# Moving one MLP tile between the score and the state products of a linear-attention output

## The reference

```python
for t in range(S):
    cur = np.einsum('bhd,bhe->bhde', u[None] * kt, vt)
    y[:, :, t] = np.einsum('bhd,bhde->bhe', rt, state + cur)
    state = wt[:, :, :, None] * state + np.einsum('bhd,bhe->bhde', kt, vt)
...
h = x @ w_in
g = np.where(h > 0.0, h, alpha * (np.exp(np.minimum(h, 0.0)) - 1.0))
x = g @ w_out
...
h = x @ w_in2
out = (h * (1.0 / (1.0 + np.exp(-1.702 * h)))) @ w_out2
```

## Time and profile before

| | |
|---|---|
| median of 3 runs | 1036.31 us (1035.52 to 1036.63) |
| profiled execution, its time | 1033.64 us |
| profiled execution, its span | 1031.5 us |
| TensorE busy | 953.8 us, 92% |
| VectorE busy | 548.6 us, 53% |
| ScalarE busy | 456.4 us, 44% |
| mean granted TensorE clock | 0.973 |
| the seven riding steps | about 90 to 573 us from the start |

### The profile page before, as it was taken

The page is one execution under the profiler, slowest core; times in us unless marked ns, Lnnn a source line. Parts: engine busy times, 40 slices in busy tenths (PEclk is TensorE's granted clock), DMA queues, the critical chain, the costliest instruction groups (busy, mean ns, idle before and its releaser), DMA issues.

```text
span 1031.5 us, 27033 instructions
## 1 busy us (share of the span) xinstructions
PE 953.8 (92%) x11872; PEld 922.7 (89%) x11872; DVE 548.6 (53%) x900; ACT 456.4 (44%) x859; POOL 54.0 (5%) x62
## 2 busy tenths in 40 slices
PE   3647999999989999999999999999999999999998
PEld 3537989888988889899888999999999999999998
DVE  7758558567477566585574443443343433443333
ACT  2343643644634635536445576333333333333332
POOL 2011000000000000000000164000000000000000
PEclk8567999999999999999999999999999999999999
DMA  6154121130130211211200651000000000000000
GB/s 167 43 142 116 25 54 48 25 87 15 31 95 7 68 51 25 54 48 24 58 22 2 216 176 44 1 24 1 23 0 24 0 23 0 23 0 24 1 24 24
DMA packets 15413, 47.29 MB, mean 46 GB/s; under 512 B 2864, under 2 KB 6832, under 8 KB 15312
## 3 DMA queue, kind: packets, MB, share of 16 engines
q1 hardware_dynamic: 12720, 38.21, 13.1%
q0 software_dynamic: 1952, 6.81, 2.1%
q10 hardware_dynamic: 640, 0.72, 0.3%
HBM read 35.71 MB, written 8.85 MB: 43 GB/s over the span
## 4 chain that ended last, share of the span: by engine, by line
PE 82%; DVE 9%; issue 4%; ACT 3%; DMA 1%; DVEq 0%; ACTq 0%
PE psum L1089 37%; PE psum L1102 34%; PE psum L941 4%; DVE blocks L667 2%; DVE arena L613 2%; PE psum L1043 1%; DVE arena L580 1%; ACT expo L411 1%; PE psum L1002 1%; PE psum L903 1%; ACT expo L409 1%; PE psum L950 1%; PE psum L1038 1%; DVE gate L713 1%; DVE x_lo L700 1%
## 5 line engine op out<-in xcount | busy, mean ns | idle before, releaser
L1089 PE MATMUL psum<-x_hi,w_split 128*128 128x384 f32 x1536 | 395.6, 338 | 1.0 <-issue 1.0
L1102 PE MATMUL psum<-g_hi,w_split 128*128 128x384 f32 x1536 | 393.2, 337 | 0.0
L1089 PE MATMUL psum<-x_lo,w_split 128*128 128x384 f32 x768 | 264.9, 345 | 21.2 <-DVE x_lo L700 19.3
L1089 PEld LDWEIGHTS psum<-x_hi,w_split 128*128 128x128 f32 x1536 | 281.9, 189 | 1.2 <-issue 1.1
L1102 PEld LDWEIGHTS psum<-g_hi,w_split 128*128 128x128 f32 x1536 | 278.5, 189 | 0.0
L1102 PE MATMUL psum<-g_lo,w_split 128*128 128x384 f32 x768 | 262.0, 341 | 0.0
L420 ACT ACTIVATE g_hi<-gate 128x384 fp32r<-128x384 f32 x256 | 134.5, 525 | 169.5 <-DVE gate L713 87.0
L718 DVE TENSOR_TENSOR g_lo<-gate,g_hi 128x384 fp32r<-128x384 f32 x256 | 142.8, 558 | 124.1 <-ACT g_hi L420 123.4
L1089 PEld LDWEIGHTS psum<-x_lo,w_split 128*128 128x128 f32 x768 | 144.9, 189 | 25.9 <-DVE x_lo L700 15.2
L711 DVE TENSOR_TENSOR gate<-expo,psum 128x384 f32<-128x384 f32 x128 | 70.9, 554 | 162.8 <-ACT expo L416 162.8
L713 DVE SCALAR_TENSOR_TENSOR gate<-expo,psum 128x384 f32<-128x384 f32 x128 | 70.9, 554 | 150.1 <-ACT expo L411 150.1
(11 more groups left out here) (64 smaller groups left out, 454.4 us busy)
## 6 DMA issues: line engine op xcount, KB each, us to landing
v_sb<-v_tokens_dram SPq DMA_DIRECT2D x8, 576.0 KB, 5.8
staging<-weights_dram POOLq DMA_DIRECT2D x11, 384.0 KB, 4.9
arena<-w_channels_dram SPq DMA_DIRECT2D x14, 288.0 KB, 4.9
arena<-k_channels_dram SPq DMA_DIRECT2D x14, 288.0 KB, 4.2
arena<-r_channels_dram SPq DMA_DIRECT2D x14, 288.0 KB, 4.7
x_scratch<-x_sb SPq DMA_DIRECT2D x7, 576.0 KB, 3.4
arena<-x_scratch SPq DMA_DIRECT2D x1, 4032.0 KB, 12.4
blocks<-weights_dram SPq DMA_DIRECT2D x9, 384.0 KB, 3.5
```

What stands on the lines that cost most here:

```text
L1089: mm = pe.matmul(hidden(f), w_tile(f, lo, m * P), xx, start=n == 0, stop=n == 3 * KT - 1)
L1102: mm = pe.matmul(acc(to, m), w_tile(f, lo, (KT + m) * P), gg, start=f == 0 and n == 0, stop=f == NF - 1 and n == 2)
```

## The change: the state products move behind down(11)

The function `outputs` gets an argument `part`. Part 0 is the score products with all waits ahead of them, part 1 the state products with theirs. In the riding steps part 0 stays where `outputs` stood, and part 1 is called behind down(11). Step 0 calls both parts in a row, as before. No product, wait or transfer is added or removed. All lines behind L1045 get higher numbers by 2, so that up's L1089 becomes L1091 and down's L1102 becomes L1104.

```diff
-                def outputs(b, i, half):
+                def outputs(b, i, half, part):
...
-                    pe.wait_ge(asm_done, i * N_ASM + N_ASM)
-                    if is_first(i):
-                        pe.wait_ge(off_done, N_OFF)
-                    else:
-                        pe.wait_ge(state_done, states_before(b, half) + N_STATE[half])
-                    pe.sem_inc(level_open, 1)
-                    for n, pair in enumerate(((4, 1), (0, 3), (2, 5))):
...
+                    if part == 0:
+                        pe.wait_ge(asm_done, i * N_ASM + N_ASM)
+                        if is_first(i):
+                            pe.wait_ge(off_done, N_OFF)
+                        else:
+                            pe.wait_ge(state_done, states_before(b, half) + N_STATE[half])
+                        pe.sem_inc(level_open, 1)
+                        for n, pair in enumerate(((4, 1), (0, 3), (2, 5))):
...
+                        return
                     if is_first(i):
                         pe.wait_ge(state_done, N_STATE[0])
                     for n, (even, odd) in enumerate((((0, 2), (1, 3)), ((4, 5), (0, 2)), ((1, 3), (4, 5)))):
...
                     unit_up(11)
-                    outputs(b, i, half)
+                    outputs(b, i, half, 0)
                     unit_down(11)
+                    outputs(b, i, half, 1)
                     unit(12)
...
-                outputs(0, 0, 0)
+                outputs(0, 0, 0, 0)
+                outputs(0, 0, 0, 1)
```

More of the change, by code:

```diff
@@ L1044, in from_state @@
                                          r[rows, a, u, c * CH:(c + 1) * CH], start=False, stop=True, skip_group_check=True)
-                    pe.wait_ge(asm_done, i * N_ASM + N_ASM)
-                    if is_first(i):
-                        pe.wait_ge(off_done, N_OFF)
-                    else:
-                        pe.wait_ge(state_done, states_before(b, half) + N_STATE[half])
-                    pe.sem_inc(level_open, 1)
-                    for n, pair in enumerate(((4, 1), (0, 3), (2, 5))):
[L1053 to L1061, removed]
+                    if part == 0:
[6 more added lines that the diff above has]
+                        for n, pair in enumerate(((4, 1), (0, 3), (2, 5))):
+                            if n == 2:
+                                pe.wait_ge(y_done, i * N_Y + 1)
+                                pe.sem_inc(level_open, 1)
+                            for u in range(U):
+                                for a in range(2):
+                                    for c in pair:
+                                        mm = from_scores(c, u, a)
+                            if n != 1:
+                                mm.then_inc(y_done, 1)
+                        return
                     if is_first(i):
```

## The result

The changed kernel takes 1038.12 us (median of 20 runs, 1034.64 to 1040.66). The kernel before took 1035.53 us beside it (20 runs, 1032.12 to 1038.59). The ratio is 1.0024 [1.0013, 1.0034], so 2.6 us more where 0.0 was forecast. 1038.12 lies inside the range of 1034.5 to 1038.6, near its upper end.

What follows compares the result with a forecast made beforehand. TensorE's up and down tiles bound the kernel, with two chains meeting at each x_lo. Terms -0.42, -0.33, +0.3, +0.15 and +0.3 us sum to 0.0, giving 1036.3 us, range 1034.5 to 1038.6.

Steps and rivals of the forecast that it cites:

- What the change does to up(14): On TensorE in riding steps, up(14) ends 0.07 us earlier per step, -0.42 us over six steps.
- (b): The wide tile down(11) itself takes 1.67 us, as before, since small products stand ahead of it in both orders.
- (c): A new change from wide to small products ahead of the state products adds 0.09 us.
- (d): The state products take 2.23 us as before, with two drains of 0.18 us in them unchanged.
- (e): up(14), now following small products, pays 0.08 us for that, as down(11) does.
- The stall that isn't in the code: TensorE's lost time in odd steps' state products, 0.33 us in step 3 and 0.70 in step 7, should go.
- The copies' shift: Output copies on ScalarE come 1.5 us later; they and work queued behind them on ScalarE and VectorE don't delay TensorE.
- The gap transfers in even steps: Later gap transfers make x_lo late in steps 2, 4, 6: 0.1 us each, ends 0 and 0.55, +0.3 in all.
- Odd steps and step 7: x_lo 0.05 us late in each of steps 1, 3, 5, +0.15 in all; in step 7 0.3 us late.
- The slow one: Rival: gap transfers keep their long form in even steps and become the bound; 1038.5 us, chance 0.2.
- Stalls that stay: Rival: step 3 keeps its 0.33 us, step 7's x_lo is about 1.0 us late; 1037.3 us, chance 0.12.
- drains worth more: Rival: changes between wide and small products are free, 0.24 us gained a step; 1033.7 us, chance 0.12.

Runs made afterwards that it cites:

- VectorE shifted: Changed kernel with 16 semaphore raises nobody waits for on VectorE ahead of step 1: 1034.36 us, ratio 0.9988.
- without transfers: Changed kernel with the small gap transfers removed, SP and POOL raising the counts at once, part of the output not computed: 1035.04 us, ratio 0.9988.
- ScalarE shifted: Changed kernel with 16 semaphore raises nobody waits for on ScalarE ahead of its step 1: 1036.55 us, ratio 1.0016.
- the first pair of experiments: x_lo made ahead of the last five tree products: on the kernel before 1028.76 us, ratio 0.9934; on the changed kernel 1038.19 us, ratio 1.0022.
- loads held back: Changed kernel with SP's loads of r and v waiting for all gap transfers of the step: 1042.47 us, ratio 1.0071.
- steps 2 to 5: Kernel before with the state products moved behind down(11) only in looped steps 2 to 5: 1037.12 us, ratio 1.0021.
- steps 2 and 4: Kernel before with the state products moved behind down(11) only in even looped steps 2 and 4: 1036.56 us, ratio 1.0013.
- the scores move too: Changed kernel with the score products also put behind down(11), both parts in a row: 1038.03 us, ratio 1.0027 to the kernel before.
- x_lo is first: Changed kernel with x_lo made on VectorE ahead of the last five tree products: 1038.19 us, ratio 1.0022 to the kernel before.
- the form with steps 1, 6 and 7: Kernel before with the state products moved behind down(11) only in written-out steps 1, 6 and 7: 1034.72 us, ratio 0.9998.

## Why the prediction missed, step by step

**What the change does to up(14): right.** Over the seven steps: (a) scores to down(11) 1.49 to 1.52 us for 1.50; state products at 3.25 to 3.28 for 3.26, which holds (b) and (c). Step 4 alone has 1.67 and 3.44. (d) is 2.24 in step 2 for 2.23; there up(14) starts 5.52 behind the scores instead of 5.67. Less 0.08 for (e) that leaves the 0.07 us a step that was taken. With no cost in the transfers the change should gain, and the ratios lean that way where they are in time: 0.9988 [0.9977, 1.0000] with VectorE shifted, 0.9988 [0.9974, 1.0002] without transfers. Neither is clear of 1.

**The stall that isn't in the code: right that it goes, too small in size.** Step 7's state products take 2.37 us and step 3's 2.28, without any "issue"; before it was 3.23 and 2.86. The 2.53 us forecast for 48 products was 0.25 us too long: 32 records a group take hardly more than the 24, 24 and 32 of an even step, which take 2.24. So steps 1 and 5, which the forecast counted as having no stall, had lost 0.3 us each as well (2.63 and 2.59 us before, 2.28 and 2.27 after). Two state groups of the changed kernel in step 7:

```profile
567.26 0.67 PE L1043 MATMUL psum<-arena,state 48*48 48x64 f32 x32
568.11 0.78 PE L1043 MATMUL psum<-arena,state 48*48 48x64 f32 x32 [0.18 <-PE psum L1043]
```

With the wide tile between, the stall is gone. That it was a block of instructions coming late stays a reading; no run varied it alone. Other "issue" entries in step 3 add up to 0.7 to 3.3 us and vary from kernel to kernel (3.2 in the changed kernel with VectorE shifted, which isn't slow), so 0.33 us on this term was below what this scatter hides. The Trainium skill (Runtime: NRT & Kernel Launch, "Instruction fetch mechanics") says that each sequencer drives its own DMA queue for its instructions and that crossing a block is mostly hidden. On the first the trace doesn't show a queue for each: VectorE's transfers and ScalarE's both stand under queue 14. With VectorE shifted, those that start at 139.1 and 212.7 us (changed kernel, profiled again) come at 116.5 and 199.9 us. With ScalarE shifted these two are within 1.2 us of their old times, as all of step 2 is, and the one at 193.4 us comes at 182.2 us. On the second, what this case adds is the cost to others: x_hi on ScalarE is held up, by a block that is VectorE's.

**The copies' shift: right.** ScalarE's first copy comes 4.97 us behind the scores instead of 3.45: 1.5 later. No run shows a cost of the later loads of r and v by themselves.

**The gap transfers in even steps: this is the step that failed.** Its words are: "I take 0.1, for a part of the overlap that may stay", with ends 0 and 0.55. In steps 4 and 6 that was right (TensorE waits 1.42 and 1.25 us against 1.33 and 1.26 before), and SP's issues did fall back to 1.78 us in all steps. In step 2 the lateness was 1.34 us. The prediction's own sign of being wrong, x_lo waiting 0.5 us or more for x_hi in an even step, came true there with 1.33 us. The row of the instruction transfer of TensorE next to the old place had been read the earlier trace rows, and the gap transfers moved away from it; what they moved towards was not looked at. It was in the trace of before: the block on queue 14 between 213.8 and 214.6 us, 1.1 us behind the last landing of the gap transfers at 212.8. That the old order missed it was luck. The upper end of 0.55 was no bound, for it held only the transfers' old form.

**What a late x_lo costs: also missing.** The forecast let a microsecond of lateness cost a microsecond. In step 2 an up(0) that came 1.35 us later brought 1.55 us more at the 1.2 GHz level.

**Odd steps and step 7: near.** TensorE's waits in steps 3 and 5 are 1.58 and 1.41 for 1.33 and 1.33, 0.25 and 0.08 us more, and in step 1 the same, 0.33 in all against 0.15 taken. Behind step 7 up(0) comes 13.30 us behind the scores instead of 13.12: 0.18 for 0.3.

**The rivals.** The slow one had the place (the gap fill), and its 1038.5 us were near 1038.12 by luck, as it had another mechanism: 0.55 us in each even step, from a long form of SP's issues. Here one step did it all, with a crossing transfer and a lost clock. Its point of decision, the spare 1.04 us, was rightly computed, and that the shift of 1.5 us uses it up is what the first pair of experiments shows. Stalls that stay, and drains worth more, are out.

## What to carry to other kernels

When a piece of work moves in time, list every transfer in the stretch it moves into, the instruction queues' among them, not only what it moves away from. A chain whose spare time falls to 0.1 us is at the mercy of a landing that varies from 1.9 to 3.2 us, so a shift that uses up spare time has a price even where the profile's typical step shows none. And read the granted clock behind each wait: here it doubled what the wait cost.

The gain here was on the other chain: making x_lo ahead of the tree gave 0.66%, and only in the order that left the outputs their spare time.

## What the runs showed of the hardware

- With VectorE's instruction transfer of 8 KB inside them, the last of SP's 24 KB transfers landed after 3.2 us instead of 1.9. Moving it by 16 instructions that do nothing on VectorE gave 1034.36 us, the same on ScalarE 1036.55 us. Why so small a block delays the landing by 1.3 us is open: the last data packet of the gap transfers had ended at 213.4, and x_hi started at 215.00.
- Waits of TensorE for x_lo of 1.13 to 1.60 us, with wide tiles around them, left the granted clock at 1.00. Behind the waits of 2.47 (loads held back), 2.62 (again), 2.68 (ScalarE shifted), 2.76, 2.89 (steps 2 to 5) and 3.01 us (steps 2 and 4) the next 3 us had 0.50 to 0.52. With 2.62 us where the scores move too it was 0.66, with 2.77 us where x_lo is first 0.61. In the form with steps 2 and 4, 0.50 stood for at least 5.6 us.
- The length of the wait doesn't decide alone. In the old order with VectorE shifted, a stall of 0.74 us between the small state products of step 7 was followed by the 1.2 GHz level:

```profile
565.39 1.23 PE L1045 MATMUL psum<-arena,state 48*48 48x64 f32 x41 [0.74 <-issue]
...
566.40:569.80 3.40, 3.40 (x23) 3.27 (x14) 1.22 (x3) 1.02 (x4) 1.08 (x3) 0.50 0.06 13
```

- Both kernels with x_lo first in the old order show the same in step 7 (stalls of 0.72 and 0.75 us), and the form with steps 1, 6 and 7 in its step 3, which isn't moved (0.59 us). With 0.74 us in step 7 the profile of the kernel before kept 1.00. What decides between them is open.
- Open: why the old order without gap transfers is 1.7 us slower than with them. Its profile has 13.5 us in the wait ahead of the riding steps instead of 11.5, but that wait is 9.2 to 13.5 us over all profiles of the study, and the profile with 9.2 us is of a slower kernel too.
